# First row block of w3 · w_out in plain fp32 from unsplit tiles, w1 and w2 loaded later

## Chip, cores and metric

One core of a Trainium2 chip runs the kernel. The metric is the device time of one execution in microseconds, lower is better; it is measured in several executions, and one more is profiled.

## What is computed

An attention step between tokens and states, then two feed-forward stages. All inputs are fp32, and the result has to have fp32 accuracy.

```python
B, H, S, Ns, D = (8, 8, 512, 32, 64)
scores = scale * x @ state.T;  a  = softmax(scores);   xread = a @ state
scores2 = scale * state @ x.T; a2 = softmax(scores2);  sread = a2 @ x
x = concat([xread, sread])      # 4608 tokens, 512 features
h = (x @ w1) * (x @ w2) @ w3    # w1, w2: 512 x 1024; w3: 1024 x 1024
x = h @ w_out                   # w_out: 1024 x 512
h = x @ w_in                    # w_in: 512 x 2048
out = (h - tanh(h)) @ w_out2    # w_out2: 2048 x 512
```

## The kernel before

TensorE multiplies fp32 numbers in one of two ways. In the **plain** way both operands are fp32. In the **split** way each operand is cut into a high and a low part of the type fp32r (ScalarE copies the tile with rounding into the high part, VectorE subtracts that from the tile for the low part), and three products hi·hi, hi·lo, lo·hi are accumulated (PASSES, three matmuls for one). Big products are split, small ones and transposes are plain.

Since w3 and w_out stand next to each other, the kernel computes their product w34 (1024 x 512) once, in the front stage, which is also where the attention is done. After that come the states' rows (stage_ys), the first feed-forward stage (stage_moe1) and the second (stage_moe2), which take most of the time.

**Front stage** (stage_front, lines 242 to 753). It goes through B = 8 batches e. In each one TensorE works in an order written out by hand (lines 717 to 743): `scores(e)` (states against tokens), `sread_turn(e - 1)`, `piece(e, 0)`, `scores_turn(e)`, `piece(e, 1)`, `a_turn(e - 1)`, `piece(e, 2)`, `a2_turn(e)`, the last piece, and `sread(e)`. Batch 0 has an order of its own, behind a warm-up of WARM = 44 transposes of an identity. The product w34 is cut into 8 row blocks r (128 rows, the `w3T` tile of r against all of `wos`), and each block into 4 pieces of two k steps, 6 matmuls of 128 x 128 x 512 in the split way. PIECES says how many of the 32 pieces stand in each batch, and they are done in order, whichever batch they fall into: piece p belongs to block p // 4. They fill TensorE's time while ScalarE and VectorE work on the softmax.

Block r of w3 is loaded into `w3r[r % 2]` (load_w3, line 332) and split by `split_w3(r)`: ScalarE's high part into `w3T` hi (line 383), then VectorE's low part over the loaded tile (line 500), which counts `w3_lo` up. The first piece of a block waits for `w3_lo`. When a block's product is done, `empty_prod(r)` splits the PSUM bank `pz[r % 2]` into w34 (lines 391 and 510). w_out is loaded as `wor` in four slices and split by `split_wo(n)` (lines 387 and 505), the low part in the place of the loaded one.

ScalarE and VectorE follow orders written out in the same way. In ScalarE's batch e (lines 460 to 480): `copy_st`, in some batches a split of w, `exp_a2`, for e = 1 `split_w3(2)`, `turn_a(e - 1)`, `exp_a`, `turn_a2`, `split_w3(e + 2)`, `copy_sr`. In VectorE's batch (lines 579 to 600): `copy_srT`, `tokens_max`, split of w, `rows_max`, `rows_sub`, `tokens_invert`, pieces(e, 1), for e = 1 `split_w3(2)`, `rows_sum`, `split_w3(e + 2)`, `rows_invert`. `rows_sub(e)` waits for `a_turn(e - 1)`, since both use the tile `a`. `sread(e)` waits for `xs(e)` and for `turn_a2(e)`.

**Loads.** All but one of the loads are issued by SyncE (SP) from one in-order queue (lines 343 to 362). xT and xs have one buffer each, so that xT(e + 1) waits for scores(e) and xs(e + 1) for sread(e). `load_w(q)` brings rows 128 q to 128 q + 127 of w1 and of w2 (2 x 512 KB). The first `split_w` waits for all four pairs, `w_in[ab] >= 16 * Q` with Q = 4 (lines 399 to 401).

**split_w(f)** (lines 398 and 517) makes the operands of `s1(f)`, the states' product with w1 and w2, which follows the eight batches; it uses a ring of WRING = 4. In ScalarE's and VectorE's batch loops:

```python
if e >= B - WRING:            # 584, 464
    split_w(e - B + WRING)
```

Of the kernel before, what the change touches and what calls it, by code (L numbers as in the profile page):

```python
# [33 lines left out]
B, H, S, D, NS = 8, 8, 512, 64, 32  # L34
# [30 lines left out]
def plain(ap):  # L65

    return ap.bitcast(F32)
# [2 lines left out]

PASSES = ((0, 0), (0, 1), (1, 0))
LAST = len(PASSES) - 1
PIECES = (4, 5, 5, 4, 4, 4, 4, 2)
WARM = 44
WRING = 4


# [164 lines left out]
def stage_front(nc, sem, room_a, room_b, room_c, room_o, small, w_at, x_rows, x_cols, state_cols, w1, w2, w3_cols, wo, aT, aT_at, w34,  # L242
# [50 lines left out]
    sT_in, xT_in, xs_in = [sem(f"sT_in{n}") for n in range(2)], sem("xT_in"), sem("xs_in")  # L293
    w_hi, w_lo = sem("w_hi"), sem("w_lo")
    w3_in, w3_hi, w3_lo = [sem(f"w3_in{n}") for n in range(2)], sem("w3_hi"), sem("w3_lo")
    wo_in, wo_hi, wo_lo = [sem(f"wo_in{n}") for n in range(NF1 // 2)], sem("wo_hi"), sem("wo_lo")
    prod_done, prod_hi, prod_lo = sem("prod_done"), sem("prod_hi"), sem("prod_lo")
    scored, st_copied, st_turned, row_max, row_sub, row_exp = (
# [32 lines left out]

    def load_w3(eng, r):

        after(eng, prod_done, r - 1)
        eng.dma_start(w3r[r % 2][:, :, :], w3_cols[r]).then_inc(w3_in[r % 2], 16)

    def sync(sp):
        wo_v = wo.rearrange("(k p) c -> p k c", p=P)

        def load_wo(n):  # L340
            sp.dma_start(wor[:, 2 * n:2 * n + 2, :], wo_v[:, 2 * n:2 * n + 2, :]).then_inc(wo_in[n], 16)

        load_w3(sp, 0)
        load_wo(0)
        load_wo(1)
        load_xT(sp, 0)
        load_wo(2)
        load_wo(3)
        load_w3(sp, 1)
        load_xs(sp, 0)  # L350
        sp.dma_start(sT[:, 1:B, :, :], state_cols[:, 1:B, :, :]).then_inc(sT_in[1], 16)
        load_xT(sp, 1)
        load_w(sp, 0)
        load_w3(sp, 2)
        load_xs(sp, 1)
        for e in range(1, B - 1):
            load_xT(sp, e + 1)
            if e < Q:
                load_w(sp, e)
            if e + 2 < NF1:  # L360
                load_w3(sp, e + 2)
            load_xs(sp, e + 1)

    def gpsimd(pool):
        pool.memset(ident[:, :], 0.0).then_inc(ident_zeroed, 1)
# [11 lines left out]

    def scalar(act):
        def split_w3(r):
            act.wait_ge(w3_in[r % 2], 16 * (r // 2 + 1))  # L380

            after(act, prod_done, r - 1)
            act.activation(w3T[0][r % 2][:, :, :], w3r[r % 2][:, :, :], ACT.Copy).then_inc(w3_hi, 1)

        def split_wo(n):
# [1 line left out]
            act.activation(wos[0][:, 2 * n:2 * n + 2, :], wor[:, 2 * n:2 * n + 2, :], ACT.Copy).then_inc(wo_hi, 1)  # L387

        def empty_prod(r):
            act.wait_ge(prod_done, r + 1)  # L390
            act.activation(w34[0][:, r, :], pz[r % 2], ACT.Copy).then_inc(prod_hi, 1)

        def pieces(e, *numbers):
# [38 lines left out]
        def turn_a(e):  # L432
            act.wait_ge(a_turned, e + 1)
            if e == 6:

                act.wait_ge(prod_done, NF1)
            for g in range(G):
                act.activation(aT[:, g, e, :], pt[g], ACT.Copy).then_inc(aT_out, 1)

# [5 lines left out]
                act.activation(sr[:, g * D:(g + 1) * D], ps[:, g * D:(g + 1) * D], ACT.Copy, scale=tinv[:, g:g + 1]).then_inc(sr_copied, 1)  # L445

        act.dma_start(sT[:, 0:1, :, :], state_cols[:, 0:1, :, :]).then_inc(sT_in[0], 16)
        split_w3(0)
        split_wo(0)
        split_wo(1)  # L450
        split_wo(2)
        copy_st(0)
        split_wo(3)
        exp_a2(0)
        split_w3(1)
        turn_a2(0)
        exp_a(0)
        pieces(0, 3)
        copy_sr(0)
        for e in range(1, B):  # L460
            copy_st(e)
            if e == 2:
                split_w3(3)
            if e >= B - WRING:
                split_w(e - B + WRING)
            pieces(e, 0)
            exp_a2(e)
            pieces(e, 1)
            if e == 1:
                split_w3(2)  # L470
            turn_a(e - 1)
            exp_a(e)
            pieces(e, 2)
            if e == B - 1:
                values.scalar_unit(act, 0, 0, pz)
            turn_a2(e)
            pieces(e, 3, 4)
            if 4 <= e + 2 < NF1:
                split_w3(e + 2)
            copy_sr(e)  # L480
        act.wait_ge(srT_copied, B)
        for k in range(KC):
            act.activation(srs[0][:, k, :], srT[:, k, :], ACT.Copy).then_inc(sr_hi, 1)
        values.scalar_unit(act, 0, 1, pz)
        for f in range(NF1):
            act.wait_ge(s1_done, f + 1)

            after(act, s1_pm, f - 1)
            act.activation(am[:, f % 2, :], bank[4 + 2 * (f % 2)][:, 0:NSTATE], ACT.Copy).then_inc(s1_am, 1)
            act.wait_ge(s1_pm, f + 1)  # L490
            act.activation(pst[0][:, f, :], pm[:, f % 2, :], ACT.Copy).then_inc(s1_hi, 1)
            if f + WRING < NF1:
                split_w(f + WRING)
            if f == 1:
                turn_a(B - 1)

    def vector(dve):
        def split_w3(r):
            dve.wait_ge(w3_hi, r + 1)
            dve.tensor_tensor(w3T[1][r % 2][:, :, :], w3r[r % 2][:, :, :], plain(w3T[0][r % 2][:, :, :]), ALU.subtract  # L500
                              ).then_inc(w3_lo, 1)

        def split_wo(n):
            dve.wait_ge(wo_hi, n + 1)
            dve.tensor_tensor(wos[1][:, 2 * n:2 * n + 2, :], wor[:, 2 * n:2 * n + 2, :], plain(wos[0][:, 2 * n:2 * n + 2, :]),
                              ALU.subtract).then_inc(wo_lo, 1)

# [55 lines left out]
            dve.wait_ge(sr_turned, e + 1)  # L563
            dve.tensor_copy(srT[:, :, e * NS:(e + 1) * NS], ps[:, W:W + P].rearrange("p (q n) -> p q n", n=NS)).then_inc(srT_copied, 1)

        split_w3(0)
        split_wo(0)
        split_wo(1)
        split_wo(2)
        tokens_max(0)  # L570
        split_wo(3)
        rows_max(0)
        rows_sub(0)
        tokens_invert(0)
        split_w3(1)
        rows_sum(0)
        pieces(0, 3)
        rows_invert(0)
        for e in range(1, B):
            copy_srT(e - 1)  # L580
            tokens_max(e)
            if e == 2:
                split_w3(3)
            if e >= B - WRING:
                split_w(e - B + WRING)
            pieces(e, 0)
            rows_max(e)
            rows_sub(e)
            tokens_invert(e)
            pieces(e, 1)  # L590
            if e == 1:
                split_w3(2)
            pieces(e, 2)
            rows_sum(e)
            if e == B - 1:
                values.vector_unit(dve, 0, 0, pz)
            pieces(e, 3, 4)
            if 4 <= e + 2 < NF1:
                split_w3(e + 2)
            rows_invert(e)  # L600
        copy_srT(B - 1)
        for k in range(KC):
            dve.wait_ge(sr_hi, k + 1)
            dve.tensor_tensor(srs[1][:, k, :], srT[:, k, :], plain(srs[0][:, k, :]), ALU.subtract).then_inc(sr_lo, 1)
        values.vector_unit(dve, 0, 1, pz)
        for f in range(NF1):
            dve.wait_ge(s1_am, f + 1)

            after(dve, s1_hi, f - 1)
            after(dve, s1_lo, f - 1)  # L610
            dve.tensor_tensor(pm[:, f % 2, :], am[:, f % 2, :], bank[5 + 2 * (f % 2)][:, 0:NSTATE], ALU.mult).then_inc(s1_pm, 1)
            dve.wait_ge(s1_hi, f + 1)
            if f == NF1 // 2:

                dve.wait_ge(a_turned, B)
            dve.tensor_tensor(pst[1][:, f, :], pm[:, f % 2, :], plain(pst[0][:, f, :]), ALU.subtract).then_inc(s1_lo, 1)
            if f + WRING < NF1:
                split_w(f + WRING)

    def tensor(pe):  # L620
# [61 lines left out]
        def sread_turn(e):  # L682
            pe.wait_ge(sr_copied, 2 * e + 2)
            pe.transpose(ps[:, W:W + P], sr[:, :], ident[:, :]).then_inc(sr_turned, 1)

        def piece(e, m):
            if m >= PIECES[e]:
                return
            p = first_piece[e] + m
            r, n = p // 4, p % 4  # L690
            if n == 0:
                pe.wait_ge(w3_lo, r + 1)

                after(pe, prod_lo, r - 1)
            if r == 0:
                pe.wait_ge(wo_lo, n + 1)
            for k in (2 * n, 2 * n + 1):
                for m, (s, t) in enumerate(PASSES):
                    mm = pe.matmul(pz[r % 2], w3T[s][r % 2][:, k, :], wos[t][:, k, :],
                                   start=k + m == 0, stop=k == NF1 - 1 and m == LAST)  # L700
            if n == 3:
                mm.then_inc(prod_done, 1)
# [12 lines left out]
            mm.then_inc(s1_done, 1)  # L715

        warm()
        piece(0, 0)
        piece(0, 1)
        scores(0)  # L720
        scores_turn(0)
        piece(0, 2)
        a2_turn(0)
        piece(0, 3)
        sread(0)
        for e in range(1, B):
            scores(e)
            sread_turn(e - 1)
            piece(e, 0)
            scores_turn(e)  # L730
            piece(e, 1)
            a_turn(e - 1)
            piece(e, 2)
            if e == B - 1:

                pe.wait_ge(prod_lo, NF1)
                values.tensor_unit(pe, 0, 0, pz)
            for n in range(3, PIECES[e] - 1):
                piece(e, n)
            a2_turn(e)  # L740
            if PIECES[e] > 3:
                piece(e, PIECES[e] - 1)
            sread(e)
# [610 lines left out]
```

## Time and profile before

| | |
|---|---|
| median of 3 runs | 1282.63 us (1282.21 to 1283.83) |
| profiled execution, its own time | 1282.33 us |
| its span | 1280.5 us |
| TensorE busy | 1259.8 us |
| VectorE busy | 774.5 us |
| ScalarE busy | 555.7 us |
| DMA | 63.77 MB, mean 50 GB/s |

The span runs from the first to the last instruction of the profiled execution, and 1.8 us of its own time lie around it. Busy times are sums of instruction durations that overlap on TensorE. The front stage is the first tenth of the span. In the profile PE is TensorE's matmuls, PEld its weight loads, DVE VectorE, ACT ScalarE, SP SyncE; the arrow in the last column names what ended the idle time before an instruction.

### The profile page before, as it was taken

The numbers are of one execution on the slowest core, as the hardware profiler recorded it, in microseconds if no ns is written. First come the engines' busy times: TensorE is split into PE (matmuls) and PEld (weight loads), VectorE is DVE, ScalarE is ACT, GpSimd is POOL, SyncE is SP. The second block draws the span as 40 slices with busy tenths as digits, with TensorE's granted clock in tenths as the row PEclk, the third lists the DMA queues.
The fourth block names the chain that finished last, engine by engine and source line by source line (L and its number), as shares of the span: only waits on it lengthen the run. The fifth ranks groups of instructions, "written<-read, shape, count | busy, mean of one in ns | idle before, by whom it ended". The sixth has DMA issues, their size and how long they took to land. (4 is left out here: it accounts for less than half of the span.)

```text
span 1280.5 us, 17462 instructions
## 1 busy us (share of the span) xinstructions
PE 1259.8 (98%) x6772; PEld 1016.6 (79%) x6772; DVE 774.5 (60%) x1268; ACT 555.7 (43%) x1035; POOL 16.0 (1%) x14
## 2 busy tenths in 40 slices
PE   9999999999999999999999999999999999999997
PEld 7768777777777777788888888888888888888886
DVE  6785244434333434678767677676676676776765
ACT  6675233323323333445444444344444444444443
POOL 0110000000000000000000000000000000000000
PEclk9999999999999999999999999999999999999999
DMA  9850200000000012212100100101001001010000
GB/s 375 315 183 1 83 1 33 34 1 34 34 1 33 34 34 115 66 50 66 50 1 17 50 9 21 37 18 49 0 16 49 3 14 49 16 41 0 8 34 17
DMA packets 17326, 63.77 MB, mean 50 GB/s; under 512 B 1904, under 2 KB 3056, under 8 KB 12656
## 3 DMA queue, kind: packets, MB, share of 16 engines
q1 hardware_dynamic: 17120, 62.86, 13.6%
q8 instruction: 41, 0.67, 0.2%
q14 instruction: 21, 0.17, 0.0%
q10 hardware_dynamic: 144, 0.07, 0.0%
HBM read 45.09 MB, written 17.83 MB: 49 GB/s over the span
## 5 line engine op out<-in xcount | busy, mean ns | idle before, releaser
L1174 ACT ACTIVATE hq<-bank 128x512 f32<-128x512 f32 (+1 forms) x144 | 82.8, 575 | 398.4 <-PE bank L1279 398.3
L1279 PE MATMUL bank<-ysp_hi,wi_lo 128*128 128x512 f32 (+1 forms) x576 | 217.2, 377 | 0.0
L1279 PE MATMUL bank<-ysp_lo,wi_hi 128*128 128x512 f32 (+1 forms) x576 | 217.2, 377 | 0.0
L1279 PE MATMUL bank<-ysp_hi,wi_hi 128*128 128x512 f32 (+1 forms) x576 | 217.2, 377 | 0.0
L1301 PE MATMUL wide<-wz_hi,gsp_hi 128*128 128x512 f32 x544 | 212.6, 391 | 3.5 <-DVE gsp_lo L1225 2.6
L1231 DVE TENSOR_TENSOR hw<-hw,hq 128x512 f32<-128x512 f32 (+1 forms) x144 | 95.5, 663 | 197.3 <-ACT hw L1179 197.3
L1301 PE MATMUL wide<-wz_hi,gsp_lo 128*128 128x512 f32 x544 | 211.8, 389 | 0.0
L1301 PE MATMUL wide<-wz_lo,gsp_hi 128*128 128x512 f32 x544 | 211.8, 389 | 0.0
L1279 PEld LDWEIGHTS bank<-ysp_hi,wi_hi 128*128 128x128 f32 x576 | 108.3, 188 | 20.6
L1279 PEld LDWEIGHTS bank<-ysp_lo,wi_hi 128*128 128x128 f32 x576 | 108.2, 188 | 20.6
L1279 PEld LDWEIGHTS bank<-ysp_hi,wi_lo 128*128 128x128 f32 x576 | 108.4, 188 | 20.1
L1301 PEld LDWEIGHTS wide<-wz_hi,gsp_hi 128*128 128x128 f32 x544 | 102.1, 188 | 25.8 <-DVE gsp_lo L1225 4.2
L1301 PEld LDWEIGHTS wide<-wz_hi,gsp_lo 128*128 128x128 f32 x544 | 102.0, 188 | 21.3
L1301 PEld LDWEIGHTS wide<-wz_lo,gsp_hi 128*128 128x128 f32 x544 | 102.2, 188 | 20.6
L1225 DVE TENSOR_TENSOR gsp_lo<-gb,gsp_hi 128x512 fp32r<-128x512 f32 (+1 forms) x144 | 95.5, 663 | 13.5 <-ACT gsp_hi L1167 0.5
L1031 PE MATMUL wide<-psp_hi,w_hi 128*128 128x512 f32 x256 | 103.3, 403 | 0.0
L1245 DVE COPY_PREDICATED gb<-far,wide 128x512 f32<-128x512 uint8 (+1 forms) x144 | 100.8, 700 | 0.1
L1031 PE MATMUL wide<-psp_hi,w_lo 128*128 128x512 f32 x256 | 100.1, 391 | 0.0
L1031 PE MATMUL wide<-psp_lo,w_hi 128*128 128x512 f32 x256 | 99.6, 389 | 0.0
L1247 DVE TENSOR_TENSOR gb<-bank,gb 128x512 f32<-128x512 f32 (+1 forms) x144 | 95.3, 662 | 5.0
L1235 DVE SCALAR_TENSOR_TENSOR gb<-hw,bank 128x512 f32<-128x512 f32 (+1 forms) x144 | 93.8, 651 | 0.0
L1167 ACT ACTIVATE gsp_hi<-gb 128x512 fp32r<-128x512 f32 (+1 forms) x144 | 86.2, 598 | 3.5 <-DVE gb L1247 3.5
(119 smaller groups left out, 1774.5 us busy)
## 6 DMA issues: line engine op xcount, KB each, us to landing
xT<-in_x_cols SPq DMA_DIRECT2D x8, 1024.0 KB, 7.5
xs<-in_x_rows SPq DMA_DIRECT2D x8, 1024.0 KB, 5.1
y_dram<-ysb SPq DMA_DIRECT2D x8, 1024.0 KB, 4.3
out<-ysb SPq DMA_DIRECT2D x8, 1024.0 KB, 4.6
yr<-y_dram SPq DMA_DIRECT2D x28, 256.0 KB, 3.8
w3r<-in_w_cols SPq DMA_DIRECT2D x8, 512.0 KB, 5.1
w_raw<-in_moe_w SPq DMA_DIRECT2D x8, 512.0 KB, 9.3
wi_raw<-in_moe_w_in SPq DMA_DIRECT2D x4, 1024.0 KB, 7.1
```

The source lines that it names most:

```text
L1031: mm = pe.matmul(py[c], w34[s][:, f, c * P:(c + 1) * P], psp[t][:, f % 2, :], start=f + m == 0, stop=f == NF1 - 1 and m == LAST)
L1167: act.activation(gsp[0][:, slot, 0:w], gb[:, slot % 2, 0:w], ACT.Copy).then_inc(g_hi, 1)
L1174: act.activation(hq[:, f % 2, 0:w], ph[f % 2][:, 0:w], ACT.Square).then_inc(sq_done, 1)
L1225: dve.tensor_tensor(gsp[1][:, slot, 0:w], g, plain(gsp[0][:, slot, 0:w]), ALU.subtract).then_inc(g_lo, 1)
L1231: dve.tensor_tensor(u, u, q, ALU.mult).then_inc(w2_done, 1)
L1235: dve.scalar_tensor_tensor(g, u, 1.0, h, ALU.add, ALU.mult).then_inc(near_done, 1)
L1245: dve.copy_predicated(g, far[:, f % 2, 0:w], pq[f % 2][:, 0:w]).then_inc(sel_done, 1)
L1247: dve.tensor_tensor(g, h, g, ALU.subtract).then_inc(g_done, 1)
L1279: mm = pe.matmul(ph[f % 2][:, 0:w], wi[s][c][:, f * P:(f + 1) * P], ysp[k][u][c][:, 0:w], start=c + m == 0, stop=c == KC - 1 and m == LAST)
L1301: mm = pe.matmul(po[j], gsp[s][:, f % 4, j * P:(j + 1) * P], wz[u][:, f, :], start=f + m == 0, stop=f == NF2 - 1 and m == LAST)
```

## The change

Row block 0 is computed by `first(n)` in plain fp32 from `w3r[0]` and `wor` as loaded, two matmuls in place of six for each quarter. So w3's block 0 is not split at all, the split of w_out's slice n waits for `first(n)`, and counts of w3_lo, w3_hi and prod_done begin with block 1. Block 0 of w3 is loaded in two halves around w_out's first slice. The warm-up has 20 transposes for 44, and the pieces are dealt out anew. The loads of w1 and w2 go behind xs(e + 1) of their batch in SP's queue, from e = 1 on, and their splits begin in batch 5 for batch 4.

```diff
-PIECES = (4, 5, 5, 4, 4, 4, 4, 2)
-WARM = 44
+PIECES = (6, 4, 4, 4, 4, 4, 4, 2)
+WARM = 20
...
     def load_w3(eng, r):
-        after(eng, prod_done, r - 1)
+        if r == 2:
+            eng.wait_ge(first_done, 4)
+        else:
+            after(eng, prod_done, r - 2)
...
-        load_w3(sp, 0)
+        load_first(0)
         load_wo(0)
+        load_first(1)
         load_wo(1)
...
         load_xT(sp, 1)
-        load_w(sp, 0)
         load_w3(sp, 2)
         load_xs(sp, 1)
         for e in range(1, B - 1):
             load_xT(sp, e + 1)
-            if e < Q:
-                load_w(sp, e)
             if e + 2 < NF1:
                 load_w3(sp, e + 2)
             load_xs(sp, e + 1)
+            if e <= Q:
+                load_w(sp, e - 1)
...
     def scalar(act):
-        split_w3(0)
         split_wo(0)
         split_wo(1)
+        copy_st(0)
         split_wo(2)
-        copy_st(0)
-        split_wo(3)
         exp_a2(0)
         split_w3(1)
         turn_a2(0)
+        split_wo(3)
         exp_a(0)
...
-            if e == 2:
-                split_w3(3)
-            if e >= B - WRING:
-                split_w(e - B + WRING)
+            if e > B - WRING:
+                split_w(e - B + WRING - 1)
...
-            if 4 <= e + 2 < NF1:
+            if e + 2 < NF1:
                 split_w3(e + 2)
...
         values.scalar_unit(act, 0, 1, pz)
+        split_w(WRING - 1)
...
     def vector(dve):
         def split_wo(n):
             dve.wait_ge(wo_hi, n + 1)
+            dve.wait_ge(first_done, n + 1)
...
-        split_w3(0)
         split_wo(0)
         split_wo(1)
+        tokens_max(0)
         split_wo(2)
-        tokens_max(0)
-        split_wo(3)
         rows_max(0)
         rows_sub(0)
+        split_w3(1)
         tokens_invert(0)
-        split_w3(1)
+        split_wo(3)
         rows_sum(0)
...
     def tensor(pe):
+        def first(n):
+            pe.wait_ge(first_in[n // 2], 16)
+            pe.wait_ge(wo_in[n], 16)
+            for k in (2 * n, 2 * n + 1):
+                mm = pe.matmul(pz[0], w3r[0][:, k, :], wor[:, k, :], start=k == 0, stop=k == NF1 - 1)
+            mm.then_inc(first_done, 1)
...
             if n == 0:
-                pe.wait_ge(w3_lo, r + 1)
+                pe.wait_ge(w3_lo, r)
                 after(pe, prod_lo, r - 1)
-            if r == 0:
+            if r == 1:
                 pe.wait_ge(wo_lo, n + 1)
...
         warm()
-        piece(0, 0)
-        piece(0, 1)
+        first(0)
+        first(1)
         scores(0)
+        first(2)
         scores_turn(0)
-        piece(0, 2)
+        first(3)
         a2_turn(0)
-        piece(0, 3)
         sread(0)
+        piece(0, 4)
+        piece(0, 5)
```

VectorE's order has the same four edits of the batch loop as ScalarE's. `if e == 1: split_w3(2)` stays where it was in both.

## Rows read from the trace of the kernel before

**Rows 1.** The page: TensorE's busy time over the whole span.

```profile
PE 1259.8 (98%) x6772; PEld 1016.6 (79%) x6772; DVE 774.5 (60%) x1268; ACT 555.7 (43%) x1035; POOL 16.0 (1%) x14
```

**Rows 2.** Windows in the warm-up: PE, PEld, DVE, ACT, POOL; clock; DMA share, GB/s.

```profile
5.00:6.00 1.00, 1.00 (x6) 1.00 (x6) 0.03 (x1) 0.94 (x1) 0.00 (x0) 1.00 1.05 387
6.00:7.00 1.00, 1.00 (x11) 1.00 (x10) 1.00 (x1) 0.81 (x1) 0.00 (x0) 1.00 1.16 461
```

**Rows 3.** Timeline, TensorE, batch 0 and scores(1): start us, duration us, what.

```profile
1.53 7.20 PE L625 MATMUL wide<-ident 128*128 128x128 f32 x44 [1.53 <-POOL ident L367]
...
8.66 0.47 PE L699 MATMUL bank<-wos_hi,w3T_hi 128*128 128x512 f32 x1
...
11.60 1.09 PE L637 MATMUL wide<-xT,sT 64*32 64x512 f32 x16
...
19.23 1.10 PE L678 MATMUL wide<-xs,a2T 128*32 128x64 f32 x64
...
20.29 1.09 PE L637 MATMUL wide<-xT,sT 64*32 64x512 f32 x16
```

**Rows 4.** DMA loads issued at 2.20, 2.71, 67.30, 68.37: us to landing.

```profile
xT<-in_x_cols SPq DMA_DIRECT2D x1, 1024.0 KB, 7.9
...
wor<-in_moe_w_out SPq DMA_DIRECT2D x1, 512.0 KB, 8.8
...
xs<-in_x_rows SPq DMA_DIRECT2D x1, 1024.0 KB, 4.9
...
xT<-in_x_cols SPq DMA_DIRECT2D x1, 1024.0 KB, 7.6
```

**Rows 5.** Groups of instructions, 0 to 130 us: busy us, mean ns, idle before.

```profile
L699 PE MATMUL bank<-wos_hi,w3T_hi 128*128 128x512 f32 x64 | 27.6, 431 | 0.0
...
L637 PE MATMUL wide<-xT,sT 64*32 64x512 f32 x128 | 8.7, 601 | 0.0
...
L510 DVE TENSOR_TENSOR w_lo<-bank,w_hi 128x512 fp32r<-128x512 f32 x8 | 5.4, 676 | 2.4 <-ACT w_hi L391 2.4
```

**Rows 6.** Timeline of batch 1: TensorE, then VectorE twice.

```profile
25.14 1.04 PE L666 MATMUL wide<-ident,a 128*128 128x128 f32 x8
...
26.28 1.22 DVE L546 TENSOR_TENSOR a<-wide,rmax 128x1024 f32<-128x1024 f32 x1 [0.74 <-PE wide L666]
...
27.70 1.20 DVE L500 TENSOR_TENSOR w3T_lo<-w3r,w3T_hi 128x1024 fp32r<-128x1024 f32 x1
```

**Rows 7.** Timeline, TensorE: first instructions of batches 2 to 7.

```profile
32.15 1.09 PE L637 MATMUL wide<-xT,sT 64*32 64x512 f32 x16
...
44.00 1.09 PE L637 MATMUL wide<-xT,sT 64*32 64x512 f32 x16
...
55.89 1.09 PE L637 MATMUL wide<-xT,sT 64*32 64x512 f32 x16
...
67.18 1.09 PE L637 MATMUL wide<-xT,sT 64*32 64x512 f32 x16
...
77.65 1.09 PE L637 MATMUL wide<-xT,sT 64*32 64x512 f32 x16
...
88.78 1.09 PE L637 MATMUL wide<-xT,sT 64*32 64x512 f32 x16
```

**Rows 8.** Timeline: ScalarE's split of w3(4), its split_w in batch 5; sread(5).

```profile
44.86 1.06 ACT L383 ACTIVATE w3T_hi<-w3r 128x1024 fp32r<-128x1024 f32 x1 [2.44 <-DMA w3r<-in_w_cols]
...
69.30 1.05 ACT L404 ACTIVATE w_hi<-w_raw 128x1024 fp32r<-128x1024 f32 x1
...
76.62 1.10 PE L678 MATMUL wide<-xs,a2T 128*32 128x64 f32 x64
```

**Rows 9.** Batch 7: TensorE's timeline at 96.89, then windows as in rows 2.

```profile
96.89 1.09 PE L113 MATMUL bank<-w_raw,sT 64*32 64x512 f32 x16 [2.25 <-DVE w_lo L510]
...
95.00:100.00 5.00, 2.78 (x24) 1.54 (x24) 4.30 (x8) 3.69 (x7) 0.00 (x0) 0.82 0.00 0
100.00:105.00 5.00, 3.21 (x83) 2.15 (x84) 1.60 (x7) 2.14 (x8) 1.91 (x1) 0.84 0.01 3
```

More of the change, by code:

```diff
@@ L295, in stage_front @@
     w3_in, w3_hi, w3_lo = [sem(f"w3_in{n}") for n in range(2)], sem("w3_hi"), sem("w3_lo")
+    first_in, first_done = [sem(f"first_in{n}") for n in range(2)], sem("first_done")
     wo_in, wo_hi, wo_lo = [sem(f"wo_in{n}") for n in range(NF1 // 2)], sem("wo_hi"), sem("wo_lo")
@@ L341, in load_wo, with load_first @@
             sp.dma_start(wor[:, 2 * n:2 * n + 2, :], wo_v[:, 2 * n:2 * n + 2, :]).then_inc(wo_in[n], 16)
-        load_w3(sp, 0)
+        def load_first(n):
+            half = slice(n * NF1 // 2, (n + 1) * NF1 // 2)
+            sp.dma_start(w3r[0][:, half, :], w3_cols[0, :, half, :]).then_inc(first_in[n], 16)
+        load_first(0)
         load_wo(0)
+        load_first(1)
         load_wo(1)
@@ L379, in split_w3 @@
         def split_w3(r):
-            act.wait_ge(w3_in[r % 2], 16 * (r // 2 + 1))
-            after(act, prod_done, r - 1)
+            act.wait_ge(w3_in[r % 2], 16 * ((r + 1) // 2))
+            if r == 2:
+                act.wait_ge(first_done, 4)
+            else:
+                after(act, prod_done, r - 2)
             act.activation(w3T[0][r % 2][:, :, :], w3r[r % 2][:, :, :], ACT.Copy).then_inc(w3_hi, 1)
@@ L389, in empty_prod @@
         def empty_prod(r):
-            act.wait_ge(prod_done, r + 1)
+            if r == 0:
+                act.wait_ge(first_done, 4)
+            else:
+                act.wait_ge(prod_done, r)
             act.activation(w34[0][:, r, :], pz[r % 2], ACT.Copy).then_inc(prod_hi, 1)
@@ L434, in turn_a @@
             if e == 6:
-                act.wait_ge(prod_done, NF1)
+                act.wait_ge(prod_done, NF1 - 1)
             for g in range(G):
@@ L498, in split_w3 @@
         def split_w3(r):
-            dve.wait_ge(w3_hi, r + 1)
+            dve.wait_ge(w3_hi, r)
             dve.tensor_tensor(w3T[1][r % 2][:, :, :], w3r[r % 2][:, :, :], plain(w3T[0][r % 2][:, :, :]), ALU.subtract
@@ L581, in vector @@
             tokens_max(e)
[L582 to L585, printed above, removed]
+            if e > B - WRING:
+                split_w(e - B + WRING - 1)
             pieces(e, 0)
@@ L597, in vector @@
             pieces(e, 3, 4)
-            if 4 <= e + 2 < NF1:
+            if e + 2 < NF1:
                 split_w3(e + 2)
@@ L605, in vector @@
         values.vector_unit(dve, 0, 1, pz)
+        split_w(WRING - 1)
         for f in range(NF1):
```

## The prediction

> **What bounds the kernel now.** I read the page first: TensorE is busy for 1259.8 us, 98% of the span [rows 1]. Whatever the front stage gains or loses in TensorE's order therefore moves all that follows by the same amount. Then I read the front stage batch by batch in the timeline. The start of scores(e) marks a batch. Batch 5, with four pieces, takes 77.65 - 67.18 = 10.47 us; batch 2, with five, 44.00 - 32.15 = 11.85 us [rows 7]. So a piece costs 1.38 us and **10.47 us is TensorE's own time for a batch of four**. Batch 1 took 32.15 - 20.29 = 11.86 us, also TensorE's own time [rows 3, 7]. Batches 3, 4 and 6, four pieces each, took 11.89, 11.29 and 11.13 us [rows 7]: they lose 1.42, 0.82 and 0.66, 2.9 us in all. What the first loss is shows in ScalarE: it sat idle for 2.44 us until block 4 of w3 had landed, and began its split only at 44.86, 0.86 us into batch 3 [rows 8]. copy_sr stands behind that split, and sread_turn behind copy_sr. The change can win at two places: the start, and these 2.9 us.
>
> **The start.** Before, TensorE warmed up for 7.20 us and began the product at 8.66 [rows 3]. What comes next is set by transfers. xT was issued at 2.20 and landed 7.9 us later, at 10.1; w_out's slice 2 at 2.71 + 8.8 = 11.5 [rows 4]. So 512 KB take 1.4 us in this full queue, and loading w3's block in halves lets slice 0 land some 0.7 us sooner, but all that lies behind both halves stays where it was.
>
> The plain product has no row of before. One matmul of the split way costs 1.38 / 6 = 0.23 us. But scores is plain, with 512 columns too: 8 matmuls in the code, 16 records in the trace, so two records for one matmul. Its eight tiles lie in different parts of the array (2 groups of rows, 4 of columns) and run side by side, so the burst is two records in a row: it lasts 1.09 us, a record 0.60, and the second one starts 0.49 behind the first at most [rows 3, 5]. The other reading: a record lasts 601 ns for 431 in the split way, and 0.23 plus that 0.17 is 0.40. From below a plain matmul costs two records of the split way, 0.46 us, from above 2 x 0.49 = 0.98. I take 2 x 0.445 = 0.89, the middle of the two readings of the scores rows, which are nearest. The block then costs 8 x 0.89 = 7.1 us for 4 x 1.38 = 5.5 before: **1.6 us more TensorE work**. The Trainium skill, "FP8 and Floating Point Precision", section TensorE Precision Notes, says that true fp32 takes four passes; by that the block would cost 5.5 x 4/3 = 7.4 us for the split way's three, an estimate, and the gain below would be 0.3 less. No row here shows a full plain tile.
>
> Step by step: first(0) begins at about 5.5, when half of w3's block and slice 0 are there, first(1) is done near 9.4, and scores(0) starts at 10.2, behind xT, for 11.60 before [rows 3]. That is 1.4 us earlier. From there to sread(0) it took 19.23 - 11.60 = 7.63 us, a chain through ScalarE's and VectorE's work. first(2) and first(3) are 0.4 longer each than the pieces in their places and first(2) waits for slice 2 until 11.5, so I add 0.2: sread(0) at 18.05. ScalarE's and VectorE's moved splits lie in waits of that chain or behind it: the split of slice 3 goes behind turn_a2(0), and with it exp_a, rows_sum and rows_invert start no earlier than before. That costs nothing, since a_turn(0) has time until batch 1's middle. Behind sread(0) come two pieces of block 1, 2.8 us, and scores(1) starts at 18.05 + 1.05 + 2.8 = 21.9, for 20.29. Then 26 of the 32 pieces are left, 28 before. **Gain at the start: 2 x 1.38 - 1.6 = 1.2 us.** Between 0.2 (plain price at its upper bound, or the late clock of rival b) and 1.6.
>
> **Batch 1, a new wait.** With PIECES = (6, 4, ...) batch 1 has pieces 6 to 9, and its third, right behind a_turn(0), is the first of block 2. It waits for w3_lo of block 2. But split_w3(2) has stayed where it was: in VectorE's order behind rows_sub(1), which itself waits for a_turn(0). Before, block 2 began two pieces and more later, as the batch's fifth. Times from batch 1's start at 20.29 [rows 3, 6]: a_turn(0) starts at +4.85 and gives way to the next piece about 0.8 later, +5.65. rows_sub starts at +5.99 and the split of w3 1.42 after it. Now empty_prod(1) stands between (block 1 is done by then), 0.68 us by its mean [rows 5]. So the split starts at +8.1 and ends at +9.3. **TensorE waits from +5.65 to +9.3: 3.65 us.** Nothing hides it: all that is queued behind, a2_turn(1), piece 9, sread(1), batch 2, moves with it. ScalarE's high part (behind exp_a2 and empty_prod) is ready before VectorE gets there, as is block 2 itself, issued now at some 16 us. Bounds: 3.4 and 3.9.
>
> **The clock.** The trace has a case of what such a pause does: TensorE sat idle for 2.25 us before 96.89, and the next two windows of 5 us show a granted clock of 0.82 and 0.84 for 1.00 [rows 9]. That is 0.18 x 5 + 0.16 x 5 = 1.7 us of full clock lost, a stretch of 3.4 us at the lower level, 1.2 GHz. A pause of 3.65 us is longer, so I expect such a stretch here. Part of it may fall into the pause itself, and there it costs nothing. Cost between 0 and 1.7; I take 1.2. The Trainium skill, "TensorE: Matmul & The Clock Gate", section "HAM oscillation", warns of the same: idle between bursts sends the clock back, and it prices the penalty as half the throttled time. By that it would be 1.7 here.
>
> **Batches 2 to 4, the load of w moved.** w1 and w2 still need 2 x 512 KB in each of four batches, now in batches 2 to 5, and right behind xs at a batch's start; xT, w3 and all else come behind. Per batch it is 3.5 MB as before. Batch 2 had them before too, and w3(4) landed at 44.86 - 32.15 = 12.7 us after its start [rows 7, 8]. But batch 2 was then 11.85 long; now it is 10.47. So block 4 lands up to 12.7 - 10.5 = 2.2 us into batch 3, 1.4 later than before. It may come some 1 us sooner, as w3(4) is asked for one piece earlier and the queue is empty when batch 2 starts. The loss was 1.42 with a landing near +0.8, so I take a loss of 1.7 in batch 3 (1.3 to 2.7), 0.2 in batch 4 (0 to 1.0), whose split_w is gone and which follows a stretched batch. Batch 2 none.
>
> **Batch 5, a wait for w.** The last pair, load_w(3), is issued only when sread(4) is done, thus at the very start of batch 5. ScalarE's split_w(0), which waits for all four pairs, stood 69.30 - 67.18 = 2.1 us into batch 5 [rows 7, 8]; it still stands there, behind copy_st(5). Before, in batch 5, xs (1 MB) was issued at 67.30 and landed 4.9 later, at +5.0; xT, the second megabyte, was issued at 68.37 and landed 7.6 later, +8.8 [rows 4]. w is the second megabyte now, issued sooner. At 1.4 us per 512 KB behind xs, it lands at +7.8, between +7.4 and +8.8. ScalarE is an in-order engine: behind split_w wait exp_a2(5), turn_a(4), exp_a(5) and turn_a2(5), and VectorE's rows_max and rows_sub behind its half of the split. Before, from split_w to sread(5) it was 76.62 - 69.30 = 7.32 us [rows 8]. In that stretch VectorE had tokens_max(5) to do, one instruction of this size, 1.2 us [rows 6], which now falls into the wait. That saves 0 to 1.2; I take 0.6. So sread(5) starts at 7.8 + 6.7 = +14.5 for +9.44, **5.0 us later**. TensorE's pieces run ahead and then it idles for about 2.7 us, so I add 0.8 for the lower clock (0 to 1.7). A late w3(6) lies under this wait. Loss in batch 5: 5.8 (4.6 to 7.7). Batch 6's loss of 0.66 goes, block 7 having had time.
>
> Batch 7 and what follows are as they were. split_w(3), now behind the states' last values, takes 1.05 us on ScalarE while s1(0) runs, and s1(3) needs it three s1 later; if that cover went, it would cost 1.05.
>
> **Sum.** Gain 1.2 and 2.9; loss 3.65 + 1.2 + 1.7 + 0.2 + 5.8 = 12.55. That is 8.5 us slower. The profiled execution took 1282.33 us, 1.8 more than its span and 0.3 below the median of the runs: 1290.8, or 1291.0 beside the median.
>
> **Rivals.**
> (a) One stall only, in batch 1. If w(3) were on time, as it would be with a queue that has drained faster than rows 4 show, the 5.8 drop to about 0.5: 1285.5. Against it: even xs alone never lands before +5.0, and w comes behind. 11%.
> (b) Late clock. The level rose in the warm-up: 6 matmuls in the window from 5 us, 11 in the next [rows 2]. With 20 transposes the warm-up ends at 1.53 + 20 x 0.164 = 4.8, before that rise, and 0.7 of idle follows. If the rise came only later, first(0) would run at half speed, 1.8 us longer, and scores(0) start 1.0 later; and if the pauses of batches 1 and 5 each cost the full 1.7, with w3 landing at the late ends, it is 1290.8 + 1.0 + 1.4 + 1.8 = 1295. 15%.
> (c) The other side: the late transfers go. What limits the front stage would be SP's queue, with w1 and w2 in front of xs and w3 in batches 0 to 3. If the new order brought each load in time and the waits in batch 1 and 5 were covered, the change would give the start's 1.2 and the 2.9: 1278.2. This decides itself at two points: w3_lo of block 2 must be there by +5.65 of batch 1, and w(3) by +2.1 of batch 5. The order of the instructions speaks against the first, the landings of rows 4 against the second. 4%.
> (d) Both waits are there, but short and overlapping with losses that were there anyway, so that the net is within 2.6: 3%.
> My own case has 67%.
>
> **Range and chances.** The sum of the lower bounds is +4.9 (gain 1.6, losses 3.4, 0, 1.3, 0, 4.6, less 2.9: 4.8), of the upper ones +14. (a) and (b) lie near these ends. 1286 to 1296 leaves out (c), (d) and half of (a), and the far part of (b). About 0.2%, 2.6 us, can be told from no change. Slower by more: 67 + 15 + 11 = 93%. Within: 3%. Faster: 4%.
>
> **What would show it.** In the profile after: a plain product of 16 records near 5.5 to 15.9; scores(0) at 10.2, scores(1) at 21.9; in batch 1 an idle TensorE of 3.65 us that ends with w3T_lo's subtraction; a clock below 1 around 30 us; in batch 5 ScalarE idle for over 5 us before its first split of w_raw, released by the transfer; scores(6) some 15 us behind scores(5). I'm wrong if piece 8 follows a_turn(0) without a gap, or if split_w(0) finds w landed.

## The result and the profile after

The changed kernel is **slower**: 1293.78 us in the median of 6 runs (1290.46 to 1296.09) against 1283.23 (1281.77 to 1283.93). The ratio is 1.0085, 95% interval 1.0074 to 1.0095. The profiled execution took 1294.0 us, its span is 1292.2, 11.7 more than before. 1291.0 was forecast, 1286 to 1296.

The page of the changed kernel, for [rows 1]:

```profile
PE 1263.6 (98%) x6740; PEld 1015.6 (79%) x6740; DVE 773.6 (60%) x1267; ACT 553.9 (43%) x1034; POOL 16.0 (1%) x14
```

TensorE is busy for 3.8 us more, the span is 11.7 longer. Most of the loss is waiting. The batches show where. The timeline of TensorE after, for [rows 3, 7]: warm-up, first(0), scores(0), sread(0), then scores of batches 1 to 7.

```profile
1.53 4.22 PE L637 MATMUL wide<-ident 128*128 128x128 f32 x20 [1.53 <-POOL ident L375]
...
5.60 1.96 PE L703 MATMUL bank<-wor,w3r 128*128 128x512 f32 x4
...
11.23 1.09 PE L649 MATMUL wide<-xT,sT 64*32 64x512 f32 x16 [0.56 <-DMA xT<-in_x_cols]
...
18.98 1.10 PE L690 MATMUL wide<-xs,a2T 128*32 128x64 f32 x64 [0.87 <-ACT a2T L440]
...
22.96 1.09 PE L649 MATMUL wide<-xT,sT 64*32 64x512 f32 x16
...
38.70 1.09 PE L649 MATMUL wide<-xT,sT 64*32 64x512 f32 x16
...
49.17 1.09 PE L649 MATMUL wide<-xT,sT 64*32 64x512 f32 x16
...
61.06 1.09 PE L649 MATMUL wide<-xT,sT 64*32 64x512 f32 x16
...
72.30 1.09 PE L649 MATMUL wide<-xT,sT 64*32 64x512 f32 x16
...
88.38 1.09 PE L649 MATMUL wide<-xT,sT 64*32 64x512 f32 x16
...
98.87 1.09 PE L649 MATMUL wide<-xT,sT 64*32 64x512 f32 x16
```

| | before, us | after | pieces before, after | lost |
|---|---|---|---|---|
| to scores(1) | 20.29 | 22.96 | 4, 6 | -0.1 |
| batch 1 | 11.86 | 15.74 | 5, 4 | 5.3 |
| batch 2 | 11.85 | 10.47 | 5, 4 | 0 |
| batch 3 | 11.89 | 11.89 | 4, 4 | 0 |
| batch 4 | 11.29 | 11.24 | 4, 4 | 0 |
| batch 5 | 10.47 | 16.08 | 4, 4 | 5.6 |
| batch 6 | 11.13 | 10.49 | 4, 4 | -0.6 |

(A piece counts 1.38 us.) scores(7) starts at 98.87 for 88.78, 10.1 later; the other 1.6 of the span come behind it, before the first matmul of s1 (116.37 for 104.71). From there to the end it is 1175.8 us in both.

**Batch 1** [rows 6]. TensorE's timeline shows a_turn(0), then the first matmul of block 2, piece 8, with the idle time before it and what ended it; VectorE's shows rows_sub(1), empty_prod(1) and the low part of block 2.

```profile
27.80 1.04 PE L678 MATMUL wide<-ident,a 128*128 128x128 f32 x8
...
32.22 0.50 PE L719 MATMUL bank<-wos_hi,w3T_hi 128*128 128x512 f32 x1 [3.38 <-DVE w3T_lo L512]
```

```profile
28.94 1.23 DVE L560 TENSOR_TENSOR a<-wide,rmax 128x1024 f32<-128x1024 f32 x1 [1.10 <-PE wide L678]
...
30.36 0.67 DVE L524 TENSOR_TENSOR w_lo<-bank,w_hi 128x512 fp32r<-128x512 f32 x1
...
30.95 1.22 DVE L512 TENSOR_TENSOR w3T_lo<-w3r,w3T_hi 128x1024 fp32r<-128x1024 f32 x1
```

TensorE sat idle for 3.38 us, released by line 512, the subtraction of the w3 split. Piece 8 starts 32.22 - 22.96 = 9.26 us into the batch.

**Batch 5** [rows 8]. ScalarE's timeline, the first split of w1 and w2:

```profile
79.86 1.06 ACT L418 ACTIVATE w_hi<-w_raw 128x1024 fp32r<-128x1024 f32 x1 [5.09 <-DMA w_raw<-in_moe_w]
```

It waited 5.09 us for the transfer. TensorE, a2_turn(5) and sread(5):

```profile
83.37 1.55 PE L669 MATMUL wide<-ident,stS 128*128 128x128 f32 x8 [3.20 <-ACT aT L452]
...
87.35 1.10 PE L690 MATMUL wide<-xs,a2T 128*32 128x64 f32 x64
```

It was idle for 3.20 us before a2_turn, and sread(5) came 15.05 us into the batch for 9.44.

**The clock** [rows 9]. Windows of the changed kernel, columns as there:

```profile
30.00:35.00 5.00, 2.78 (x8) 2.15 (x9) 3.26 (x6) 1.47 (x3) 0.00 (x0) 0.76 0.12 46
85.00:90.00 5.00, 5.00 (x89) 3.05 (x89) 3.55 (x6) 3.52 (x7) 0.61 (x1) 0.78 0.14 25
105.00:110.00 5.00, 3.02 (x24) 1.75 (x24) 4.10 (x7) 3.52 (x6) 0.00 (x0) 0.77 0.00 0
110.00:115.00 5.00, 4.25 (x83) 2.09 (x81) 0.74 (x3) 1.19 (x4) 1.91 (x1) 0.55 0.00 0
```

The granted clock falls behind both pauses to the lower of its two levels, 1.2 GHz, and in batch 7 the low stretch is longer than before: 0.23 x 5 + 0.45 x 5 = 3.4 us of full clock lost for 1.7. TensorE's order in batch 7 was not changed, and it is idle for 2.25 us before L113 in both kernels; this is where the last 1.6 us went.

### The profile page after: what moved, and what is told of

The parts are those of the page before. It is cut to its first block and busy times, and to the rows that moved or that the text cites. A ratio compares the mean times of both kernels' runs of the same rounds, so it can differ in the third digit from the quotient of the medians.

```text
span 1292.2 us, 17405 instructions
## 1 busy us (share of the span) xinstructions
PE 1263.6 (98%) x6740; PEld 1015.6 (79%) x6740; DVE 773.6 (60%) x1267; ACT 553.9 (43%) x1034; POOL 16.0 (1%) x14
```

## Experiments

All times are medians, each beside runs of the kernel before on the same chip (1282.8 to 1282.9). "After" is 1293.8.

**e1: the split of w3's block 2 sooner.**

```diff
-            if e == 1:
-                split_w3(2)
...
         pieces(0, 3)
         copy_sr(0)
+        split_w3(2)
```

(VectorE: behind rows_invert(0).)

> The changed kernel with one move: the split of w3's block 2 goes from the middle of batch 1 to the end of batch 0 on ScalarE (behind copy_sr) and VectorE (behind rows_invert). Theory A (batch 1's 15.74 us are TensorE's 10.47 plus a wait for that split, 3.3 us, and the low clock behind it, 1.7 to 2): batch 1 falls to 10.5, no low clock in it, and the whole to 1293.8 - 5.2 = 1288.6. Rival B (the plain product and its loads cost the time, the wait is only where it shows): scores(2) comes less than 1 us earlier and the whole stays over 1292.5.

Measured: 1288.29 us, ratio 1.0040 (1.0027 to 1.0053). Theory A's total, and no low stretch is left in batch 1. But the batch took 11.70, not 10.5: a new loss of 1.2. GpSimd's rows_scale(0) and VectorE's split of block 2, in the timelines of e1:

```profile
22.78 1.92 POOL L380 TENSOR_TENSOR a<-a,rinv 128x1024 f32<-128x1024 f32 x1 [21.31 <-DVE rinv L573]
...
23.09 2.68 DVE L511 TENSOR_TENSOR w3T_lo<-w3r,w3T_hi 128x1024 fp32r<-128x1024 f32 x1 [0.40 <-ACT w3T_hi L394]
```

The subtraction takes 2.68 us for 1.22, while rows_scale runs. e8 tests that.

**e2: w1 and w2 one batch sooner.**

```diff
         load_xs(sp, 1)
+        load_w(sp, 0)
...
-            if e <= Q:
-                load_w(sp, e - 1)
+            if e < Q:
+                load_w(sp, e)
```

> The changed kernel with each pair of loads of w1 and w2 issued one batch sooner, at the same place of SP's queue (behind xs). Theory A (batch 5's 16.08 us are 10.47 plus ScalarE's wait for the last pair and its low clock): batch 5 falls to 10.5 to 11.5 and the whole to 1293.8 - 5.1 = 1288.7; batch 1 keeps its 15.7. Rival B (the wait in ScalarE would have been hidden, batch 5 is long because of the late w3 block): batch 5 stays over 14, the whole over 1292.

Measured: 1288.68 us, ratio 1.0040 (1.0024 to 1.0055). Batch 5 takes 11.21. Rival B is out. Batch 1 gave something unasked. TensorE's timeline (piece 8) and a window of e2:

```profile
31.48 0.50 PE L720 MATMUL bank<-wos_hi,w3T_hi 128*128 128x512 f32 x1 [3.38 <-DVE w3T_lo L513]
...
30.00:35.00 5.00, 3.52 (x19) 3.00 (x20) 2.56 (x3) 2.03 (x4) 0.00 (x0) 1.00 0.16 63
```

The same pause of 3.38 us, and here the clock stayed at 1.00; batch 1 took 14.17 us, not 15.74. So the wait costs 3.7 and the low clock, where it comes, 1.6 more.

**e3: both.** The edits of e1 and e2.

> Both moves together, the early split of block 2 and the loads of w1 and w2 one batch sooner. Theory A (two independent waits, each with its clock): 1293.8 - 5.2 - 5.1 = 1283.5, within 1.5 of the kernel before. Rival C (they overlap or another wait takes over): over 1286.

Measured: 1285.53 us (1282.35 to 1287.85), ratio 1.0014 (1.0004 to 1.0024). The two repairs give 8.3 us together, of 5.5 + 5.1 = 10.6 that each gave alone, so rival C has a part in it: 2.0 over the expectation. Batches 1 to 6 take 11.72, 11.32, 12.22, 11.56, 11.84 and 10.48. Part of the rest is w3's blocks, which now land late for the batches that have become shorter: ScalarE waited 7.3 us for them in four splits. Batch 1 has e1's slow subtraction again, 2.82 us.

**e4: the early split, and w1 and w2 between w3 and xs.**

```diff
             if e + 2 < NF1:
                 load_w3(sp, e + 2)
-            load_xs(sp, e + 1)
             if e <= Q:
                 load_w(sp, e - 1)
+            load_xs(sp, e + 1)
```

> The early split of block 2, and the pair of w1 and w2 between w3(e + 2) and xs(e + 1) in SP's queue, so issued about 5 us into batches 1 to 4, behind xT and w3. Theory A with its second part (the 1.4 and 0.8 us that batches 3 and 4 lose come from w3 landing behind w in the same batch): all batches 1 to 6 at 10.5 to 10.8, scores(7) at 23.0 + 6 x 10.5 = 86 for 88.8 before, the whole at 1280 to 1281, faster than the kernel before by 2 to 3. Rival D (the queue is full whatever the order): batches 2 to 5 still lose 2 us together, the whole at 1282.5 to 1284.

Measured: 1283.44 us, ratio 1.0003 (0.9994 to 1.0012), 2.4 over the upper end of the expectation. Batches 2 and 4 take 10.48, but 3 and 5 still 11.79 and 11.99. TensorE's sread_turn in these two, from the timeline of e4:

```profile
46.67 0.33 PE L694 MATMUL wide<-ident,sr 128*128 128x128 f32 x1 [1.21 <-ACT sr L459]
...
68.62 0.33 PE L694 MATMUL wide<-ident,sr 128*128 128x128 f32 x1 [0.89 <-ACT sr L459]
```

It waits for copy_sr, behind the late split of w3 on ScalarE. Moving w1 and w2 out of w3's way was not enough, and rival D's numbers came true: batches 2 to 5 lose 2.8 us together. Whether the queue alone is to blame is what e9 asks.

**e5 and e12: the plain block alone.** The kernel before with first(n), its loads and the splits behind it; PIECES and w1, w2 as before. e5 has the warm-up of 44, e12 of 20. The diff is e5's against the changed kernel.

```diff
-PIECES = (6, 4, 4, 4, 4, 4, 4, 2)
-WARM = 20
+PIECES = (4, 5, 5, 4, 4, 4, 4, 2)
+WARM = 44
```

> The kernel before with the plain first block alone: PIECES, the warm-up of 44 and the loads and splits of w1 and w2 as before; block 0 plain, its loads in halves, the splits of w_out behind it. The prediction's step for the start gives scores(1) 1.2 us sooner and the whole 1281.4; the trace of the changed kernel (scores(1) at 22.96 with two pieces, 2.8 us, more done) gives 20.2, so 0.1 sooner, and the whole at 1282.7, within 0.5 of the kernel before. Rival (the plain block is the loss): over 1284.

> As e5 (plain first block alone, pieces and loads of w1 and w2 as before) with the warm-up of 20. scores(0) starts near 10.6 and scores(1) near 19.4, for 11.60 and 20.29 before and 12.61 and 21.27 in e5: a gain of 0.9 at the start. Batches 1 to 4 keep what e5 lost there (12.9, 12.7, 11.4 and 11.9 for 11.9, 11.9, 11.9 and 11.3, block 3's split at the end of batch 1 waiting for its load): the whole 2 us under e5, 1284.5 to 1285. If e5's loss in batches 1 and 2 came from its late start, they return to 11.9 and the whole is 1282.

Measured: e5 1286.94 us, ratio 1.0032 (1.0020 to 1.0044); e12 1286.89, ratio 1.0028 (1.0018 to 1.0038). Both slower than before, and my expectation for e5 was wrong by 4. The rival's number, over 1284, came true, but the traces put the loss elsewhere than in the plain product. In e5 the long warm-up held first(0) up, until 9.08, and scores(1) starts at 21.27, 1.0 later than before. In e12 scores(0) starts at 10.41, 1.2 sooner than before, but scores(1) came only at 20.43: TensorE waited 1.19 us at its start, until xT(1) had landed at 20.34 (20.20 before). And then e12 waits for copy_sr in batches 2 and 4. TensorE's sread_turn in these two, from the timeline of e12:

```profile
35.68 0.33 PE L695 MATMUL wide<-ident,sr 128*128 128x128 f32 x1 [2.31 <-ACT sr L460]
...
60.11 0.33 PE L695 MATMUL wide<-ident,sr 128*128 128x128 f32 x1 [1.98 <-ACT sr L460]
```

So in the old order of loads the earlier start gave nothing: w3's blocks 3 and 4 landed at 34.14 and 45.50 for 33.96 and 44.84 before, and their splits (block 3's now at the end of batch 1) hold copy_sr up. I had expected a gain in e12 of 2 over e5; it was given back there. e5's profiled execution (1284.54, no low clock before its end) was also its fastest run, 2.4 under the median, so its batches show less than the whole loss.

**e7: the pause of batch 1 filled.**

```diff
             a_turn(e - 1)
+            if e == 1:
+                pe.wait_ge(prod_lo, 1)
+                for n in range(30):
+                    pe.transpose(pz[0][:, 0:P], ident[:, :], ident[:, :])
```

> The changed kernel with 30 transposes of the identity into the free bank, between a_turn(0) and the piece that waits in batch 1; they do no work, they fill 2.9 of the 3.3 us of the pause. If the low clock in that batch comes from the pause, there is no low stretch there: batch 1 takes 14.1 to 14.3 us in place of 15.7 and the whole is 1.0 to 1.6 faster than the changed kernel, 1292.4. If the low stretch has another cause, batch 1 stays at 15.7. The early kernels so far showed one run of the same pause without a low stretch (14.17 us), so the mean gain may be under 1.6.

Measured: 1290.77 us, ratio 1.0068 (1.0053 to 1.0084), 2.6 less over the kernel before than the changed kernel is. Batch 1 takes 14.15 and no stretch of the profiled execution is low before its end. That fits, but e2's unfilled pause had no low stretch either, so one profile more doesn't show that the filling did it. Batch 3 takes 13.10 us in it for 11.89, so a part of what batch 1 gained was lost again. How often the pause brings the clock down stays open.

**e8: the split of block 2 away from rows_scale.** As e4, with split_w3(2) in batch 1 behind copy_st(1) and tokens_max(1).

> As e4 (pair of w1 and w2 between w3 and xs), but the split of block 2 stands in batch 1 behind copy_st and tokens_max, not at the end of batch 0. In e4 VectorE's half took 2.79 us for 1.22 while GpSimd's rows_scale(0) ran, and batch 1 11.68 us. Theory: the two engines slow one another, and away from rows_scale the split takes 1.22 and batch 1 10.5, the whole 1.2 less than e4, 1282.2. Rival: the split is slow because of something else in that place (the DMA writing w3r): it takes over 2 us again.

Measured: 1282.62 us (1280.09 to 1285.81), ratio 0.9998 (0.9986 to 1.0011), 0.8 under e4 for 1.2 expected. GpSimd's rows_scale(0) and VectorE's split of block 2 in e8:

```profile
22.61 1.92 POOL L380 TENSOR_TENSOR a<-a,rinv 128x1024 f32<-128x1024 f32 x1 [21.14 <-DVE rinv L574]
...
25.82 1.22 DVE L512 TENSOR_TENSOR w3T_lo<-w3r,w3T_hi 128x1024 fp32r<-128x1024 f32 x1
```

1.22 us, and batch 1 takes 10.48. rows_scale had ended at 24.53. Batches 3 to 5 still take 11.50, 10.78 and 12.30.

**e9: all splits of w3 ahead.**

```diff
             copy_st(e)
-            if e > B - WRING:
-                split_w(e - B + WRING - 1)
+            if e + 1 < NF1:
+                split_w3(e + 1)
+            else:
+                split_w(2)
...
-            if e + 2 < NF1:
-                split_w3(e + 2)
+            if 5 <= e < B - 1:
+                split_w(e - 5)
             copy_sr(e)
```

(The same on VectorE; `if e == 1: split_w3(2)` is gone in both, and w1 and w2 are loaded as in e4.)

> As e8, with all splits of w3's blocks from block 2 on moved from the end of batch e - 2 to the start of batch e - 1 (behind copy_st and tokens_max), and the splits of w1 and w2 in their place at the ends of batches 5 and 6. So a w3 block that lands late holds up neither copy_sr nor rows_invert. Theory: the 1.2 to 1.4 us that batches 3 and 5 still lose in e4 are that; all batches 1 to 6 take 10.5, scores(7) starts at 22.2 + 62.8 = 85.0 for 88.8 before, and the whole is 1279 to 1279.5, ratio 0.997. Rival: something else paces them (VectorE's chain), then batches 5 and 6 take over 11 us and the whole is 1281 or more.

Measured: 1280.42 us (1278.03 to 1281.25), ratio 0.9980 (0.9971 to 0.9989), **faster than before**. All six batches take 10.48 or 10.49. TensorE's timeline, scores(1) and scores(7), and a window of e9:

```profile
22.38 1.09 PE L649 MATMUL wide<-xT,sT 64*32 64x512 f32 x16
...
85.29 1.09 PE L649 MATMUL wide<-xT,sT 64*32 64x512 f32 x16
...
95.00:100.00 5.00, 4.27 (x87) 2.98 (x85) 1.73 (x4) 2.39 (x6) 1.91 (x1) 0.50 0.00 0
```

scores(7) starts at 85.29, 3.5 sooner than before. From there to the first matmul of s1 it took 17.44 us for 15.93, at the low clock, so 1.5 of the 3.5 were lost again. Against e8 only the places of the splits differ, of w3's and of those of w1 and w2; the two were not moved one at a time.

**e10: block 0 in one load.** As e9, with `load_first(0)` for all of w3's block 0 and no second half.

> As e9, but block 0 of w3 comes in one load of 512 KB, not in two halves around w_out's first slice. If the halves cost the queue time (in the changed kernel w_out's slice 1 landed at 8.6 and xT at 11.1, for 7.6 and 10.1 before), slice 1 lands near 7.6, scores(0) starts near 10.1 for 10.5 to 11.2, and the whole gains up to 0.5 on e9. If they cost nothing, first(0) starts 0.6 later, scores(0) within 0.2 of e9's 10.6, and the whole is the same.

Measured: 1277.68 us (1277.63 to 1278.64), ratio 0.9962 (0.9948 to 0.9976), the best of all, 5.2 under the kernel before. w_out's slice 1 and xT in the changed kernel (issued at 2.19 and 2.67), and then, the same two lines in both, in e9 (issued as there) and in e10 (1.68 and 2.19):

```profile
wor<-in_moe_w_out SPq DMA_DIRECT2D x1, 512.0 KB, 6.4
...
xT<-in_x_cols SPq DMA_DIRECT2D x1, 1024.0 KB, 8.4
```

```profile
wor<-in_moe_w_out SPq DMA_DIRECT2D x1, 512.0 KB, 5.8
...
xT<-in_x_cols SPq DMA_DIRECT2D x1, 1024.0 KB, 7.8
```

In e9 and e10 the time from issue to landing is the same, and in e10 both are issued 0.5 us sooner, as SP's queue has one load less: xT lands at 10.02 for 10.48. Whether the issue alone does it is not shown. The halves are also moved in smaller rows, and in the window from 3 to 4 us e9 moved 274 GB/s, e10 420. The changed kernel's profiled execution had 0.6 more at both. scores(0), and the same rows of e10 as of e9:

```profile
10.16 1.09 PE L647 MATMUL wide<-xT,sT 64*32 64x512 f32 x16 [0.17 <-DMA xT<-in_x_cols]
...
21.87 1.09 PE L647 MATMUL wide<-xT,sT 64*32 64x512 f32 x16
...
84.78 1.09 PE L647 MATMUL wide<-xT,sT 64*32 64x512 f32 x16
...
95.00:100.00 5.00, 3.60 (x84) 2.10 (x82) 1.74 (x5) 2.00 (x6) 1.91 (x1) 0.73 0.00 0
```

scores(7) is 0.5 sooner than in e9; the other 2 us of the medians' difference are not shown by batches 1 to 6. In the profiled executions e9 had twice the low stretch of e10 in batch 7. The mean granted clocks of all runs point the same way, 0.998 or 0.999 in e10's five, 0.996 to 0.999 in e9's eleven.

**e11: e9 with the warm-up of 44.**

> As e9, with the warm-up of 44 transposes. They end near 8.9, so first(0) starts there and not at 5.6; first(1) behind it, scores(0) near 12.6 as in e5, 2 us later than in e9, and the whole is 1.5 to 2 us slower than e9, 1282.2. If the first product were not what scores(0) waits for, it would be the same as e9.

Measured: 1280.07 us, ratio 0.9981 (0.9971 to 0.9990), no different from e9, and the expectation was wrong: scores(0) starts 1.2 later than in e9, not 2, and scores(1) at 23.24, 0.9 later, but in the profiled execution batch 7's low stretch was 3.4 and not 6.8 us.

**e13: the kernel before with the warm-up of 20.**

> The kernel before with the warm-up of 20 alone. It ends near 5.7, the split product can begin at 8.6 as before, since the splits are not ready sooner. If a pause of 2.9 us there sends the clock down, or keeps it from rising, the first pieces run at 1.2 GHz and scores(1) starts 0.5 to 1.7 late: 1283.3 to 1284.5. If not, the kernel is the same as before: the long warm-up was needed only to bridge the splits.

Measured: 1287.53 us, ratio 1.0035 (1.0023 to 1.0048), worse than expected. TensorE's timeline of e13, the warm-up and, with their length at the lower clock, one of the first product's matmuls:

```profile
1.53 4.53 PE L625 MATMUL wide<-ident 128*128 128x128 f32 x20 [1.53 <-POOL ident L367]
...
10.04 0.63 PE L699 MATMUL bank<-wos_hi,w3T_hi 128*128 128x512 f32 x1
```

0.63 us for 0.47 in the same place before [rows 3]. The windows print a granted clock of 1.00 for these first microseconds, where the trace has no entry yet; the first one, of the full clock, begins at 13.92 in e13 and at 6.03 in the kernel before. In the low stretch of the changed kernel's batch 1 a matmul of this kind took 0.63 too. So I read it as the lower clock through the first pieces. scores(0) starts at 14.00 for 11.60, scores(1) 2.4 later than before; the rest of the 4.6 is not explained (in the profiled execution 3.2 us are lost behind the front stage, where the code is the same). In the kernel before the long warm-up bridges the time of the splits. With the plain block, which starts at 5.6, 20 transposes are enough: in e7, e8 and e12 the first entry came only at 7.60, 6.38 and 7.35, and scores(0) started at 10.41 to 10.49 all the same, behind xT.

## Why the prediction was right

The direction, the time and both waits were as forecast. 8.5 us slower were forecast; the spans differ by 11.7. The 3.2 between them are 1.1 at the start, 0.4 in batch 1, 0.3 in batches 3 and 4, -0.2 in batch 5 and 1.6 in batch 7. The waits were worked out from rows. What they do to the clock was picked between 0 and 1.7 and came out near, which was partly luck: in e2 the same wait had no low clock behind it. Step by step:

- **The start**: 1.2 us of gain was forecast, 0.1 came, just under the lower bound. The plain product was priced right, as its group shows (16 records, 0.45 apart in the timeline: 12.59 to 14.38 for two matmuls, 1.79 us for 1.78):

```profile
L703 PE MATMUL bank<-wor,w3r 128*128 128x512 f32 x16 | 7.7, 607 | 1.4 <-DMA wor<-in_moe_w_out 1.4
```

  The failed step is "all that lies behind both halves stays where it was". xT landed at 11.1, not 10.1. Of that 0.5 goes with the second half, as e9 and e10 show. The rest is in the changed kernel's profiled execution alone: in the seven other kernels with the same start (e1 to e4, e7 to e9) scores(1) starts at 22.18 to 22.38, so 0.7 to 0.9 are gained. In e10, where the block comes in one load, scores(0) starts at 10.16 and scores(1) at 21.87, for 10.2 and 21.9 forecast: the 1.2 are there. From scores(0) on, 22.96 - 11.23 = 11.73 us was as worked out (21.9 - 10.2).
- **Batch 1**: piece 8 at +9.3 forecast, +9.26 measured. e1 removes the wait, and 4.0 us of the batch and 5.5 of the whole go; e8 brings the batch to 10.48. The low clock cost 1.6 (e2 against the changed kernel), 1.2 forecast, and in e2 nothing. The Trainium skill ("TensorE: Matmul & The Clock Gate", "HAM oscillation") has idle between bursts bring the clock down; the changed kernel agrees, e2 with the same pause doesn't.
- **Batches 3 and 4**: losses of 1.7 and 0.2 forecast, 1.42 and 0.77 measured, together 0.3 more. Block 4 landed at 50.03, 0.86 into batch 3, no later than before (44.84, 0.84 into it), so the loss was the same 1.42; block 5 landed at 61.26, 0.2 into batch 4, for 0.3 ahead of it before. e4, with w1 and w2 out of w3's way, only moves the loss (0 in batch 4, 1.5 in batch 5); e9, with the splits of w3 where they hold up no copy_sr, removes it, though some of those blocks land late there too (block 5 at 54.71, 0.9 into batch 4).
- **Batch 5**: w forecast at +7.8, the split began at 79.86 - 72.30 = +7.56; loss 5.8 forecast, 5.6 measured. e2 removes 4.9 of it. The row at 69.30 that the prediction calls split_w(0) is split_w(1); split_w(0) stood in batch 4 of the kernel before. The sum doesn't change by that, as both stand behind copy_st. From the split to sread(5) it took 87.35 - 79.86 = 7.49 us, and 84.87 - 78.00 = 6.87 in e7, where the clock stayed full: so 6.87 for the 6.7 forecast, and 0.6 for the lower clock, forecast 0.8.
- **What was not foreseen**: 1.6 us in batch 7, where TensorE's order is the same. The clock there depends on more than the pause, which is 2.25 us in both. The prediction had "Batch 7 and what follows are as they were".
- **Rivals.** (a) is out, as w(3) was late by 5.09 us. Of (b), the late rise at the start didn't come in the profiled execution, where first(0) took 1.96 us as first(2) did. (c), the other side, fell as told: both its points failed. Yet e10 comes near what it described, 1278.2 forecast for a kernel in which all comes in time, 1277.7 measured. Its scores(7) is 4.0 sooner than before: 1.2 from the start, and 2.9 that batches 3, 4 and 6 lost before. The 1.2 are the change's own; two waits, both removable, and the second half of a load hid them. The 2.9 come with e9's order of loads and splits. Whether that order gives them with block 0 split as before is not shown, as no run has it.

## What to carry to other kernels

When pieces of filler work are dealt out anew, look for the first one that needs an operand prepared inside the same batch, and place that preparation by the new due time, ahead of what waits for this engine. A load moved "one batch later" in an in-order queue is later by what it then stands behind: count from the event that releases it to its first use. A step that can be late should not stand in front of one that the critical engine waits for: here the loads came first (e1 to e4, 4.9 us), and then, where reordering them gave no more, moving the splits behind copy_sr and copy_st gave another 2 or so (e8 to e9).

## What was unexpected of the hardware

- VectorE's tensor_tensor of 128 x 1024 took 2.68 us in e1 and 2.79 in e4 where it overlapped GpSimd's tensor_tensor, 1.22 in e8. In e1, GpSimd ends at 22.78 + 1.92 = 24.70; with 1.22 behind it that is 25.92, and the instruction ended at 25.77. The Trainium skill, "SBUF — State Buffer", section "SBUF: two separate sides", says that the two engines share a pair of ports, and that a VectorE instruction with two SBUF inputs and a GpSimd one that reads SBUF block each other for the whole instruction. The trace agrees to 0.2 us. e8 alone would not show this, since it moved the split away from all else in that place. But e3 has it a third time (2.82 us), and wherever VectorE's tiny tensor_scalar of 128 x 2 starts inside GpSimd's instruction, in these 14 traces, it is never done before that ends. In the changed kernel it took 0.73 us for 0.17 and ended at 54.87, GpSimd's at 54.85:

```profile
52.93 1.92 POOL L380 TENSOR_TENSOR a<-a,rinv 128x1024 f32<-128x1024 f32 x1 [11.26 <-DVE rinv L574]
...
54.14 0.73 DVE L542 TENSOR_SCALAR tbias<-tmax 128x2 f32<-128x2 f32 x1
```

- A pause of 3.38 us before piece 8 was followed by a clock of 0.76 in one kernel and 1.00 in another. Batch 7 has the same pause of 2.25 us in all 14 kernels profiled. The clock stayed full there in four (e1, e5, e7, e8); in eight it was low for 3.4 us, which takes 1.7 us of full clock, and in two (the changed kernel and e9) for 6.8, which takes 3.4. The changed kernel's runs spread over 5.6 us. The clock may be a part of that, and a ratio from single runs would be worth little here.
- Splitting one load in two made xT, two loads behind it, land 0.46 us later in one pair of profiles (10.48 for 10.02), about what one issue takes in SP's queue (0.47).
